# Turning attention probabilities by DMA in two 16-bit planes instead of on TensorE

## What is computed

```python
# attention, 8 batches, 8 heads, 576 rows, head size 64; k and v are averaged over groups of 8 rows (72 keys)
scores = q @ mean8(k).T / 8;  attn = softmax(scores);  x = attn @ mean8(v)      # -> x: 4608 tokens x 512
# dense layers
h = x @ w_in;  g = max(h, 0) + alpha * min(h, 0);  y = g @ w_out                # 512 -> 2048 -> 512
# each token goes to one of 8 experts, chosen by cosine to expert_emb, with gate softmax(logits)[best]
out = gate * (relu(y @ w1[e]) @ w2[e])                                         # 512 -> 1024 -> 512
```

## Time and profile before

| | |
|---|---|
| median of 3 runs | 1438.87 us (1436.43 to 1439.27) |
| the profiled execution, its own time | 1435.18 us |
| its span, first to last instruction | 1433.5 us |
| mean granted clock of TensorE | 0.996 |
| busy: PE, DVE, ACT, POOL | 99%, 55%, 42%, 48% |
| tiles 0 to 7 end at about | 830 us |

### The profile page before, as it was taken

One profiled execution on the slowest core, in us unless ns is written; L12 is line 12 of the kernel. 1 busy time (PEld: TensorE's weight loads), 2 busy tenths in 40 slices (PEclk: granted clock), 3 DMA queues, 4 the chain that ended last, 5 costly groups with the idle time before them and its releaser, 6 DMA issues.

```text
span 1433.5 us, 21529 instructions
## 1 busy us (share of the span) xinstructions
PE 1415.5 (99%) x7469; PEld 1166.3 (81%) x7469; DVE 794.9 (55%) x1498; ACT 606.1 (42%) x938; POOL 686.3 (48%) x613
## 2 busy tenths in 40 slices
PE   8999999999999999999999999999999999999997
PEld 7888888888888888888888888888888878887876
DVE  7656677676776767766666576680002810056660
ACT  5333332222232232232322222544676666766664
POOL 4552244253253352352232243475666766678773
PEclk9999999999999999999999999999999999999999
DMA  8544131131131230221110122354333963469641
GB/s 251 166 116 155 39 100 62 26 115 45 46 95 44 56 115 30 71 68 30 60 45 15 38 88 60 110 175 128 89 87 89 218 185 94 87 143 248 146 115 27
DMA packets 145478, 138.90 MB, mean 97 GB/s; under 512 B 87900, under 2 KB 104284, under 8 KB 145248
## 3 DMA queue, kind: packets, MB, share of 16 engines
q1 hardware_dynamic: 59200, 99.20, 22.1%
q10 hardware_dynamic: 78144, 19.41, 8.5%
q0 software_dynamic: 8032, 18.93, 4.2%
HBM read 92.34 MB, written 29.43 MB: 85 GB/s over the span
## 4 chain that ended last, share of the span: by engine, by line
PE 91%; DVE 4%; ACT 2%; DMA 1%; issue 1%; POOL 1%; SPq 0%; ACTq 0%; DVEq 0%; POOLq 0%
PE y_ps L837 26%; PE h_ps L821 25%; PE y_ps L977 15%; PE y_ps L943 15%; PE h_ps L781 3%; PE step_ps L740 2%; PE step_ps L760 2%; PE h_ps L955 1%; DVE weight_parts L1264 1%; DMA y_rows<-g_full 1%; DVE weight_parts L1259 1%; DVE rank_in_list L1204 0%; ACT L1431 0%; DMA y_rows<-in_k 0%; DVE shared L1054 0%
## 5 line engine op out<-in xcount | busy, mean ns | idle before, releaser
L1775 POOL TENSOR_TENSOR g_lo<-g_full,g_hi 128x512 fp32r<-128x512 f32 x144 | 193.1, 1341 | 514.9 <-ACT g_hi L1474 514.9
L821 PE MATMUL h_ps<-x_hi_in,weight_parts 128*128 128x512 f32 x1144 | 376.2, 392 | 0.0
L837 PE MATMUL y_ps<-weight_parts,g_hi 128*128 128x512 f32 x1152 | 359.6, 393 | 0.3 <-POOL g_lo L1775 0.3
L1474 ACT ACTIVATE g_hi<-g_full 128x512 fp32r<-128x512 f32 x144 | 91.1, 632 | 517.0 <-PE y_ps L837 413.7
L821 PEld LDWEIGHTS h_ps<-x_hi_in,weight_parts 128*128 128x128 f32 x1144 | 214.8, 188 | 43.8
L837 PEld LDWEIGHTS y_ps<-weight_parts,g_hi 128*128 128x128 f32 x1152 | 213.1, 188 | 45.7 <-POOL g_lo L1775 0.7
L943 PE MATMUL y_ps<-weight_parts,x_hi_in 128*128 (+1 forms) x1032 | 242.1, 390 | 1.3 <-DVE weight_parts L1264 0.7
L943 PEld LDWEIGHTS y_ps<-weight_parts,x_hi_in 128*128 128x128 f32 x1032 | 193.2, 188 | 42.3 <-issue 2.5
L837 PE MATMUL y_ps<-weight_parts,g_lo 128*128 128x512 f32 x576 | 224.6, 390 | 0.0
L821 PE MATMUL h_ps<-x_lo_in,weight_parts 128*128 128x512 f32 x572 | 222.8, 390 | 0.0
L1131 DVE TENSOR_SCALAR g_full<-h_ps,alpha 128x512 f32<-128x512 f32 x144 | 107.5, 747 | 194.7 <-PE h_ps L821 192.3
(11 more groups left out here) (231 smaller groups left out, 1763.8 us busy)
## 6 DMA issues: line engine op xcount, KB each, us to landing
shared<-in_w SPq DMA_DIRECT2D x8, 2048.0 KB, 10.0
emb_all<-in_w SPq DMA_DIRECT2D x8, 2048.0 KB, 9.3
y_dram<-y_rows SPq DMA_DIRECT2D x9, 1024.0 KB, 4.3
shared<-in_q SPq DMA_DIRECT2D x34, 256.0 KB, 2.9
shared<-in_v SPq DMA_DIRECT2D x29, 288.0 KB
x_dram<-shared SPq DMA_DIRECT2D x32, 256.0 KB, 3.2
y_rows<-x_dram SPq DMA_DIRECT2D x32, 256.0 KB, 3.4
shared<-in_k SPq DMA_DIRECT2D x26, 288.0 KB, 2.8
```

The costliest lines, as they stand in the source:

```text
L821: mm = pe.matmul(h_ps[:, f % 2, :], w[:, k, f * P:(f + 1) * P], x[:, k, :], start=(n == 0), stop=(n == 3 * DC - 1))
L837: mm = pe.matmul(y_ps[:, j, :], a[:, f % 2, j * P:(j + 1) * P], w[:, f, :], start=(f == 0 and n == 0), stop=(f == FC - 1 and n == 2))
L1474: act.activation(gh[:, f % 2, :], g_full[:, f % 2, :], ACT.Copy).then_inc(gh_done, 1)
L1775: pool.tensor_tensor(gl[:, f % 2, :], g_full[:, f % 2, :], gh[:, f % 2, :].bitcast(F32), ALU.subtract).then_inc(gl_done, 1)
```

## The change

For steps 8 to 35 (`TURN = 8`) PE no longer turns the probabilities and ScalarE no longer copies them out of PSUM. Instead ScalarE takes the low and the high 16 bits of each value apart, one plane at a time, into the second buffer of `prob` (8 heads, 72 of 128 columns each), issues a DMA transpose of 128x1024 16-bit values for each, and joins the turned planes in `probt`. Plane 0 lands in `xo`, plane 1 in `kt`, the buffer of keys. With f the slot in which step s was scored: part and issue of plane 0 in slot f + 1, part and issue of plane 1 and the join of plane 0 in slot f + 2, the join of plane 1 in slot f + 3, ahead of `x_out`. The steps use only the first buffer of `prob`, so `shift(s)` waits until both planes of s - 1 are parted. `exps(s)` of these steps stands ahead of `g_hi` now.

Since `kt` is taken between slots f + 2 and f + 3, the keys' loads are moved: in tiles 1 to 5 SP issues them in slots 6, 9 and 12, behind `store_x` (and, in slot 12, behind `load_x`), and in slot 15 behind a wait for the join. VectorE sums them in slots 7, 10 and 13 and in slot 0 of the next tile. Tile 0 stays as it was. The order of `load_v`'s is kept, but in slot 12 it is behind the keys' load.

```diff
+TURN = 2 * FIRST
-            return prob[:, s % 2, :, :]
+            return prob[:, s % 2 if s < TURN else 0, :, :]
...
+            if i == 0 and f in (7, 9, 11, 13):
+                return PAIRS * 2 + (f - 7) // 2
+            if 1 <= i <= BATCH - 3 and f in (7, 10, 13):
+                return PAIRS * (i + 2) + (f - 7) // 3
+            if 2 <= i <= BATCH - 2 and f == 0:
+                return PAIRS * (i + 1) + PAIRS - 1
...
+        plane = prob[:, 1, :, :].rearrange("q h n -> q (h n)").bitcast(U16)[:, 0:HEADS * P]
+        planes_t = [x.bitcast(U16)[:, 0:HEADS * QB] for x in (xo.rearrange("p c n -> p (c n)"), kt)]
...
+                    elif i <= BATCH - 3:
+                        if f in (6, 9, 12):
+                            load_k(PAIRS * (i + 2) + (f - 6) // 3)
+                        elif f == FC - 1:
+                            sp.wait_ge(plane_joined, 2 * (last_step(i + 1) + 2 - TURN))
+                            load_k(PAIRS * (i + 2) + PAIRS - 1)
...
+                if s < TURN:
+                    pe.wait_ge(turned_copied, s + 1)
+                else:
+                    pe.wait_ge(plane_joined, 2 * (s - TURN + 1))
...
-                        turn_probs(late)
+                        if late < TURN:
+                            turn_probs(late)
...
+                if s > TURN:
+                    dve.wait_ge(plane_parted, 2 * (s - TURN))
...
+            def turn_plane(s, w):
+                m = s - TURN
+                if w == 0:
+                    act.wait_ge(normed, norms(s))
+                    if m == 0:
+                        act.wait_ge(turned, TURN)
+                    act.wait_ge(stored, 16 * (s - FIRST))
+                if 2 * m + w:
+                    act.wait_ge(plane_turned, 16 * (2 * m + w))
+                bits = prob_at(s).bitcast(U16).rearrange("q h (n w) -> q h n w", w=2)
+                act.activation(plane.rearrange("q (h n) -> q h n", h=HEADS)[:, :, 0:KEYS], bits[:, :, :, w],
+                               ACT.Copy).then_inc(plane_parted, 1)
+                act.wait_ge(plane_parted, 2 * m + w + 1)
+                act.dma_start(out=planes_t[w].rearrange("p (h n) -> p h n", n=QB), in_=plane,
+                              transpose=True).then_inc(plane_turned, 16)
+
+            def join_plane(s, w):
+                m = s - TURN
+                act.wait_ge(plane_turned, 16 * (2 * m + w + 1))
+                if w == 0:
+                    act.wait_ge(av_done, s)
+                bits = probt.bitcast(U16).rearrange("p (n w) -> p n w", w=2)
+                act.activation(bits[:, :, w], planes_t[w][0:KEYS, :], ACT.Copy).then_inc(plane_joined, 1)
...
+                    s = plane_step(i, f, 1)
+                    if s is not None:
+                        turn_plane(s, 0)
+                    s = plane_step(i, f, 2)
+                    if s is not None:
+                        act.wait_ge(k_summed, k_summed_at(i, f - 1) if f else k_summed_at(i - 1, FC - 1))
+                        turn_plane(s, 1)
+                        join_plane(s, 0)
+                    s = plane_step(i, f, 3)
+                    if s is not None:
+                        join_plane(s, 1)
...
+                    s = score_step(i, f)
+                    if s is not None and s >= TURN:
+                        exps(s)
                     g_hi(i, f)
-                    s = score_step(i, f)
-                    if s is not None:
+                    if s is not None and s < TURN:
                         exps(s)
```

More of the change, by code:

```diff
@@ L348, in stages @@
         turned, turned_copied = sem("turned"), sem("turned_copied")
+        plane_parted, plane_turned, plane_joined = sem("plane_parted"), sem("plane_turned"), sem("plane_joined")
         av_done, x_done = sem("av_done"), sem("x_done")
@@ L518, in score_step, with plane_step, k_summed_at @@
             return s + 1 if s is not None and s + 1 < STEPS else None
+        scored_at = {FC * i + f: score_step(i, f) for i in range(NT) for f in range(FC)
+                     if score_step(i, f) is not None}
+        def plane_step(i, f, behind):
+            s = scored_at.get(FC * i + f - behind)
+            return s if s is not None and s >= TURN else None
+        def k_summed_at(i, f):
+            return 1 + max([n for n in (k_at(a, g) for a in range(i + 1) for g in range(FC) if (a, g) <= (i, f))
+                            if n is not None])
         def sum_step(i, f):
@@ L536, in k_at @@
                 return 2 * PAIRS - 1
-            if i <= BATCH - 3 and f in (7, 9, 11, 13):
-                return PAIRS * (i + 2) + (f - 7) // 2
+            if i == 0 and f in (7, 9, 11, 13):
[4 more added lines that the diff above has]
+                return PAIRS * (i + 1) + PAIRS - 1
             return None
@@ L630, in tile @@
                             load_x(i + 1)
-                    n = k_at(i, f)
-                    if n is not None and n + 1 < BATCH * PAIRS:
-                        load_k(n + 1)
+                    if i == 0:
+                        n = k_at(i, f)
+                        if n is not None and n + 1 < 3 * PAIRS:
+                            load_k(n + 1)
+                    elif i <= BATCH - 3:
[4 more added lines that the diff above has]
+                            load_k(PAIRS * (i + 2) + PAIRS - 1)
                     n = v_at(i, f)
@@ L731, in scores @@
                     pe.wait_ge(shifted, whole(s - 1))
-                    pe.wait_ge(turned_copied, s)
+                    pe.wait_ge(turned_copied, min(s, TURN))
                 out = scores_at(s)
@@ L770, in values @@
                     pe.wait_ge(v_pooled, v_pool_count(n))
-                pe.wait_ge(turned_copied, s + 1)
+                if s < TURN:
+                    pe.wait_ge(turned_copied, s + 1)
+                else:
+                    pe.wait_ge(plane_joined, 2 * (s - TURN + 1))
                 if 2 <= s < FIRST:
@@ L863, in ranks @@
                 pe.wait_ge(router_step, NSTEP * i + C_CHOSEN)
-                pe.wait_ge(turned_copied, last_step(min(i + 2, NT - 1)) + 1)
+                pe.wait_ge(shifted, whole(min(last_step(i + 2) + 1, STEPS - 1)))
                 pe.matmul(r_ps[:, 0:TB, :], c["before"][:, :], chosen[:, :, :], start=True, stop=False,
@@ L902, in turn_x @@
                     pe.wait_ge(x_done, STEPS)
-                    pe.wait_ge(turned_copied, STEPS)
+                    pe.wait_ge(turned_copied, TURN)
                 for k in range(DC):
@@ L1078, in shift @@
                 dve.wait_ge(maxed, s + 1)
-                if s >= FIRST:
+                if s > TURN:
+                    dve.wait_ge(plane_parted, 2 * (s - TURN))
+                elif s >= FIRST:
                     dve.wait_ge(turned, s - 1)
@@ L1461, in x_out @@
                     act.wait_ge(stored, 16 * (s - FIRST))
+                if s >= TURN:
+                    act.wait_ge(plane_joined, 2 * (s - TURN) + 1)
                 act.activation(xo[:, :, :], by_pair, ACT.Copy).then_inc(x_done, 1)
@@ L1631, in tile @@
                             w_hi(n)
+                    s = plane_step(i, f, 1)
[9 more added lines that the diff above has]
+                        join_plane(s, 1)
                     s = value_step(i, f)
                     if s is not None:
-                        copy_turned(s)
+                        if s < TURN:
+                            copy_turned(s)
                         x_out(s, (f + 1) % 2)
```

## The result

| | before | after |
|---|---|---|
| median, 4 runs each on one chip | 1438.09 us (1436.43 to 1439.27) | 1461.75 us (1452.47 to 1463.21) |
| profiled span | 1433.5 us | 1458.8 us |
| mean granted clock | 0.996 | 0.986 |

The ratio is 1.0152, 95% interval 1.0108 to 1.0196. The kernel became slower by about 1.5%. The forecast was a gain, 1434.5 us, and the time lies above its range.

A forecast was written before the change was run, and what follows sets the result against it. PE, busy 1415.5 of 1433.5 us, was taken to bound the kernel. 24.4 - 6.1 - 0.2 - 13.5 - 0.25 = 4.4 us gained gave 1430.8 us for the profiled execution, 1434.5 against the median; range 1424 to 1445.

The forecast's parts named there:

- What leaves PE: Steps 8 to 35: eight transposes leave PE in each of 28 steps, 0.87 us a step, 24.4 us gained.
- The steps' own way: Parts, transposes and joins before a step's values: plane 1 joined at 463.42, PE wanting the values at 463.45.
- The seven waits in slot 12: Steps scored in slot 9: join 1 stands behind root(), PE waits 0.88 us before values; cost 6.1 us.
- PE does not wait, with nothing to spare: Steps scored in slots 3 and 6, 14 of them: join 1 is just in time, each keeps its 0.87 us.
- Rival C: Slower: both DMA legs exceed 3.1 us, join 1 late in slots 6 and 9; up to 1454 us; chance 0.2.
- The moved key loads: Slot 12, tiles 1 to 5: late keys hold PE before ranks 2.7 us each, 13.5 us in all (4.5 to 19).
- Small things: Minor effects: g_lo late at the end of tile 0, 0.25 us; k_summed wait, slot 13's transpose and transposes' traffic given no cost.
- The end of tile 0: Slot 15: step 8's part and issue stand ahead of x_hi and g_hi, g_lo about 0.25 us too late for layer2.
- that step has slots to spare: Slot 13: the first transpose is behind GpSimd's values, but the step has time, so no cost was given.
- rival B: Keys don't hold PE, so the 13.5 us cost goes: 17.9 us gained, 1421 us; chance 0.15.
- A: The forecast itself, 1431 to 1438 us; chance 0.45.
- D: No measurable change: keys late by 3.8 us in tiles 1 to 5, 19 us in all, 1439 to 1440 us; chance 0.2.

The follow-up runs named there:

- the waits are out: The late-planes kernel with root() in slot 10, squares paired in slots 6 and 9, and a small transpose in slot 0 of tile 0: 1415.91 us.
- the moves alone: The kernel before with only the keys' loads and sums moved as in the change, PE still turning all probabilities: 1459.49 us.
- PE was kept busy: The changed kernel with 44 transposes that nobody reads put on PE ahead of ranks in tiles 1 to 5: 1454.95 us.
- the planes made late: The planes-alone kernel, with planes of steps scored at a tile's end made in slots 0 to 2 of the next tile: 1428.27 us.
- keys-first kernel: The changed kernel with the keys' load of slot 12 issued ahead of store_x and the x loads in tiles 1 to 5: 1437.34 us.
- the first two kernels: The keys-first kernel, 1437.34 us, and the changed kernel with router_choose ahead of the keys' sum in slot 13, 1438.76 us.
- planes alone: The changed kernel with plane 1 in the step's own query buffer, keys loaded and summed as in the kernel before: 1442.52 us.
- root earlier: The keys-first kernel with root() in slot 10 instead of 11: 1440.41 us.

## Why the prediction was wrong

**What leaves PE: right.** 24.4 us was the term. PE has 224 instructions less, tile 7, which has no low clock and only the wait of slot 12 (0.82 us), is 96.45 us long from ranks to ranks instead of 99.06 (2.6 shorter, as predicted), and once the waits are out the kernel gains 21.

**The steps' own way: right in its costs, too tight in its margin.** Parts take 0.68 us (0.67 taken), joins 1.36, issues 1.25. The seven waits in slot 12 are 0.82 to 1.02 us against 0.88: 6.2 as predicted. "PE does not wait, with nothing to spare" in slots 6 and 9 failed in 4 of 14 steps, 3.1 us. Tile 5 shows one; these rows are ScalarE's timeline, a leg of tile 3 first, then that of tile 5:

```profile
382.72 1.25 ACTq L1502 DMA_TRANSPOSE shared<-shared  x1
...
385.85 0.68 ACT L1499 ACTIVATE shared<-shared 128x576 uint16<-128x576 uint16 x1 [0.54 <-DMA shared<-shared]
...
572.87 1.25 ACTq L1502 DMA_TRANSPOSE shared<-shared  x1
...
577.51 0.69 ACT L1499 ACTIVATE shared<-shared 128x576 uint16<-128x576 uint16 x1 [2.66 <-DMA shared<-shared]
```

A leg of 3.1 us, and one of 4.6. Rival C said this for all 14 steps; it came in 4, and C was not the cause of the loss. Its formula, 2(d - 3.1) - 1.07, counts two long legs, and here the first alone was long: 3.9, 4.0, 4.6 and 3.9 us in tiles 2, 4, 5 and 6, and 3.0 to 3.1 for the second. Beside the medians, of which the forecast took the lower one, rows 7 show landings of up to 10.6 and 10.9 us. What made these legs long wasn't tested.

**The moved key loads: the step that failed.** "Cost 416.4 - 413.68 = 2.7 us" for each of five tiles, 13.5, with 19 as its upper bound. Measured 22.2, 4.4 per tile. The place, the chain and the five tiles were right, the sign of the term too; the landing was mis-sized. Predicted 6.4 us after the first x issue, it was 7.3 in tile 1 with the moves alone and 8.35 (209.40 to 217.75) with the planes. I had added transfers one behind the other at 0.9 us per 256 KB from a tile with nothing beside them. Here a load of values is issued at 212.59, behind the keys but before they are there, and the first of the step's transposes at 214.42 (tile 1). The moves-only kernel has its waits without any plane, 16.8 us, and with the planes they are 1.1 us a tile longer; how much of the rest is due to the values' load is not shown.

**What the sum did not have: the clock.** The sum priced a wait of PE at its own length and nothing behind it. A PE that stood for 3.7 to 4.8 us came back at 1.2 GHz for 3.1 to 5.6 us: 9.6 us by the rows, and behind `ranks` all of it returned when PE was kept busy. Together with the term above this is most of the error: 22.2 - 13.5 + 9.6 = 18.3 us. Between the forecast for the profiled execution and the one after it are 1461.15 - 1430.8 = 30.4 us (27 between the medians). Of the rest 3.1 are slots 6 and 9, 1.6 tile 0, 2.1 are not followed, and 4.8 are the experts' part.

**Small things: two of them were not.** The end of tile 0 cost 1.81 us instead of 0.25, since the first transpose, issued at 122.54, took 2.69 us to issue and 9.9 to land:

```profile
L1502 ACTq DMA_TRANSPOSE shared<-shared x56: 1247/1249/2694, 122.5 to 817.9; - x56
...
DMA to landing us min/median/max: 3.0/3.1/9.9
```

Being the kernel's first doesn't explain it. SP had issued a load of 2048 KB 1.2 us ahead of it, which took 10.1 us. With the planes made late, the kernel's first transpose is issued once that load has landed, and it takes 5.2 us, as those at the start of the tiles behind it do (5.2 to 6.1, beside a store of y). The rows are SP's in the kernel after, then ScalarE's and the landing with late planes:

```profile
121.31 0.38 SPq L674 DMA_DIRECT2D emb_all<-in_emb  x1
...
131.33 2.13 ACTq L1496 DMA_TRANSPOSE shared<-shared  x1
...
DMA to landing us min/median/max: 5.2/5.2/5.2
```

And "that step has slots to spare", said of slots 13 to 15: true for its values, but not for `g_hi` behind it in ScalarE's list. This wait was named at the end as what would make the prediction wrong and was in no term. With tile 0's part it is 8 to 13 us as soon as the keys no longer hold PE, so rival B, 1421 us once the keys are in place, was wrong as well: the keys-first kernel is B's condition, and it gave 1437.

**The rivals.** A: the mechanism held, its size did not. B: refuted by the first two kernels. C: in part, see above. D had the sign of the trouble (the keys later than forecast) and stopped at 3.8 us; tiles 1 to 4 each exceeded it.

## What to carry to other kernels

A load that is put behind others in a queue doesn't land at the sum of their lone durations; bound it from above with everything else that is in flight there, and let no instruction that PE waits for stand behind it. Price a stop of PE of some 3 us or more with the clock behind it: 1.4 to 2.6 us each here. Shorter ones are uncertain: behind one of 2.60 us nothing was lost, but behind ones of 2.55 us (planes alone, tile 3) and 1.91 us (root earlier, tile 1) the clock fell. Where an engine waits for a DMA inside a list, ask for each instruction behind it, not only for the step served, when it is needed: removing the largest wait only showed the next one. A transpose that lands in 3.1 us alone took up to 9.1 beside loads, so move it away from them first.

## What the runs showed of the hardware

- A DMA transpose of 128x1024 16-bit values landed after a median of 3.1 us and held ScalarE's queue for 1.25. Issued 1.2 us behind a load of 2048 KB it took 9.9 us and held the queue for 2.69; beside the loads of x and values it took 4.3 to 6.0 us with 2.8 to 3.9 us between the first x load and it (keys-first), and 7.6 to 9.1 with 1.6 to 1.7 us (root earlier).
- Behind stops of PE of 2.8 to 4.8 us the low clock cost 1.4 to 2.6 us each; it was back at 1.00 3.1 to 5.6 us after PE took up its work. Behind one of 2.60 us it cost nothing, and behind ones of 2.55 and 1.91 us in other kernels it fell.
- The granted clock also fell where PE had hardly stopped: at the passage to the experts in five of ten kernels, for 1.6 to 3.9 us, and twice in the kernel with PE kept busy, behind waits of 0.82 and 0.88 us.
- The 288 KB of keys landed 5.8 to 6.6 us after their issue behind four loads of x, and alone a median of 2.8.
